# Softmax reciprocals spread through a transpose and transfers from DRAM instead of small matmuls, with the value products dealt out one key tile at a time

## The reference

```python
scores = scale * np.matmul(q, k.transpose(0, 1, 3, 2))
thresh = np.max(scores, axis=-1, keepdims=True) - tau
scores = np.where(scores >= thresh, scores, -1000000000.0)
scores = scores - np.max(scores, axis=-1, keepdims=True)
attn = np.exp(scores)
attn = attn / (np.sum(attn, axis=-1, keepdims=True) + 1e-09)
x = np.matmul(attn, v)                     # then laid out as [tokens, 512]
h = x @ w_in;   x = (h * np.tanh(softplus(h))) @ w_out
h = x @ w_in2;  x = (h * np.clip(h + 3, 0, 6) / 6) @ w_out2
```

## Time and profile before

| | us |
|---|---|
| median of 3 runs (1115.53 to 1116.26) | 1115.55 |
| the profiled execution's own time | 1116.74 |
| its span | 1115.0 |
| PE busy | 1098.8 (99%) |
| DVE busy | 423.6 (38%) |
| ACT busy | 489.9 (44%) |
| POOL busy | 263.5 (24%) |

### The profile page before, as it was taken

The page is one execution under the profiler, slowest core; times in us unless marked ns, Lnnn a source line. Parts: engine busy times, 40 slices in busy tenths (PEclk is TensorE's granted clock), DMA queues, the critical chain, the costliest instruction groups (busy, mean ns, idle before and its releaser), DMA issues.

```text
span 1115.0 us, 15233 instructions
## 1 busy us (share of the span) xinstructions
PE 1098.8 (99%) x6064; PEld 880.3 (79%) x6064; DVE 423.6 (38%) x903; ACT 489.9 (44%) x882; POOL 263.5 (24%) x179
## 2 busy tenths in 40 slices
PE   6999999999999999999999999999999999999998
PEld 5767676767668888889988888888888888888897
DVE  6878887878831211112121112123223223222222
ACT  5778787877743332223232234442233233232232
POOL 6686558556621300000000015430000000000000
PEclk9999999999999999999999999999999999999999
DMA  7432223223022000000000022300010010010010
GB/s 221 132 108 65 77 74 97 65 66 96 11 76 76 1 1 1 1 1 1 1 1 1 19 75 96 96 18 1 1 38 1 1 38 0 1 39 1 1 39 20
DMA packets 42488, 46.09 MB, mean 41 GB/s; under 512 B 3504, under 2 KB 30128, under 8 KB 42416
## 3 DMA queue, kind: packets, MB, share of 16 engines
q1 hardware_dynamic: 42416, 45.10, 13.6%
HBM read 40.37 MB, written 4.72 MB: 40 GB/s over the span
## 4 chain that ended last, share of the span: by engine, by line
PE 97%; DVE 1%; ACT 1%; issue 1%; DMA 0%; SPq 0%; DVEq 0%
PE banks L489 35%; PE banks L462 12%; PE banks L464 12%; PE banks L463 12%; PE banks L409 8%; PE banks L356 7%; PE banks L368 5%; PE banks L364 3%; PE banks L389 2%; DVE probs L709 0%; DVE neg_max L725 0%; ACT exps L572 0%; DMA q_raw<-qT 0%; ACT probsT L537 0%; DVE totals L741 0%
## 5 line engine op out<-in xcount | busy, mean ns | idle before, releaser
L770 DVE SCALAR_TENSOR_TENSOR g_low<-gate,g_high 128x512 fp32r<-128x512 f32 (+1 forms) x160 | 102.7, 642 | 473.2 <-ACT g_high L645 473.2
L462 PE MATMUL banks<-x_low,w_in_high 128*128 128x512 f32 (+1 forms) x640 | 235.9, 369 | 0.0
L463 PE MATMUL banks<-x_high,w_in_low 128*128 128x512 f32 (+1 forms) x640 | 235.5, 368 | 0.0
L464 PE MATMUL banks<-x_high,w_in_high 128*128 128x512 f32 (+1 forms) x640 | 235.5, 368 | 0.0
L645 ACT ACTIVATE g_high<-gate 128x512 fp32r<-128x512 f32 (+1 forms) x160 | 94.3, 589 | 309.6 <-PE banks L489 309.1
L462 PEld LDWEIGHTS banks<-x_low,w_in_high 128*128 128x128 f32 x640 | 120.6, 188 | 21.2 <-issue 0.6
L463 PEld LDWEIGHTS banks<-x_high,w_in_low 128*128 128x128 f32 x640 | 120.6, 188 | 20.5
L464 PEld LDWEIGHTS banks<-x_high,w_in_high 128*128 128x128 f32 x640 | 120.7, 189 | 20.0
L725 DVE TENSOR_REDUCE neg_max<-banks 128x1 f32<-128x576 f32 x144 | 108.7, 755 | 50.3 <-PE banks L356 50.1
L489 PE MATMUL banks<-g_low,w_out_high 128*128 128x512 f32 (+1 forms) x320 | 118.0, 369 | 0.8 <-issue 0.8
L489 PE MATMUL banks<-g_high,w_out_low 128*128 128x512 f32 (+1 forms) x320 | 117.8, 368 | 0.0
(11 more groups left out here) (59 smaller groups left out, 1430.1 us busy)
## 6 DMA issues: line engine op xcount, KB each, us to landing
q_raw<-qT SPq DMA_DIRECT2D x64, 144.0 KB, 2.8
k_raw<-kT SPq DMA_DIRECT2D x64, 144.0 KB, 2.8
w_in_raw<-w_in SPq DMA_DIRECT2D x16, 512.0 KB, 4.3
w_out_raw<-w_out SPq DMA_DIRECT2D x16, 512.0 KB, 4.7
out<-x SPq DMA_DIRECT2D x18, 256.0 KB, 2.9
values<-v SPq DMA_DIRECT2D x16, 256.0 KB, 3.1
values<-v SPq DMA_DIRECT2D x16, 32.0 KB, 2.8
tau_in<-tau SPq DMA_DIRECT2D x1, 0.5 KB, 2.8
```

Of the source, the lines that this page charges most:

```text
L462: nc.tensor.matmul(bank, w_in_high[:, t, cols], low, start=(t == 0), stop=False)
L463: nc.tensor.matmul(bank, w_in_low[:, t, cols], high, start=False, stop=False)
L464: mm = nc.tensor.matmul(bank, w_in_high[:, t, cols], high, start=False, stop=(t == KT - 1))
L770: nc.vector.scalar_tensor_tensor(out=g_low[:, f % 2, 0:width], in0=gate[:, f % 2, 0:width], scalar=1 / 6 if layer_of(c) else 1.0, in1=f32( ...
```

## The change

The spreading matmuls and their copies are gone. In their place PE transposes the pair's 128 x 9 reciprocals once, at `i == 2` (`turn_recips`); ACT copies the 9 x 128 result to `recip_rows` (`keep_recips`); SP stores this to a DRAM row, waits until it has landed, and reads it back in three transfers that lay it out over 64 partitions each (`spread_recips`). DVE's two multiplications wait for these (`spread_loaded`). The key tiles of the value products are dealt to more steps (`part0`, `part1`), DVE's multiplications stand behind `weigh`, and the second is at `i == 2`. The end of the attention is written out by hand.

```diff
+            def spread_recips(pair):
+
+                sp.wait_ge(recip_rows_kept, pair + 1)
+                row = recip_dram[pair % 2]
+                sp.dma_start(row.rearrange("(t p) -> t p", p=P), recip_rows[:, :]).then_inc(recips_stored, 16)
+                sp.wait_ge(recips_stored, 16 * (pair + 1))
+
+                after(sp, x_ready, 2 * pair)
+                sp.dma_start(spread[0:DH, :], row[0:SEQ].partition_broadcast(DH)).then_inc(spread_loaded, 16)
+                sp.dma_start(spread[DH:P, 0:MAIN * P], row[SEQ + TAIL:2 * SEQ].partition_broadcast(DH)).then_inc(spread_loaded, 16)
+                sp.dma_start(spread[DH:P, MAIN * P:SEQ], row[SEQ:SEQ + TAIL].partition_broadcast(DH)).then_inc(spread_loaded, 16)
...
             for k in range(HEADS_IT):
                 load_head(1, k)
+            spread_recips(0)
 
             for it in range(2, ITS):
                 for k in range(HEADS_IT):
                     load_head(it, k)
+                    if k == 1:
+                        spread_recips(2 * it - 3)
                     if k % 2 == 1:
                         load_values(it - 1, k // 2)
+                spread_recips(2 * it - 2)
+            spread_recips(PAIRS - 3)
             for b in range(PAIRS_IT):
                 load_values(ITS - 1, b)
+            spread_recips(PAIRS - 2)
...
                 if g == EARLY_PIECES:
+                    spread_recips(PAIRS - 1)
...
+                    if half == 0 and i == 3:
+
+                        after(pe, recip_rows_kept, t // PAIR_TILES)
...
-            def spread_sums(pair, b, u):
-
-                if u == 0:
-                    pe.wait_ge(recips_ready, pair + 1)
+            def turn_recips(pair, b):
+
+                pe.wait_ge(recips_ready, pair + 1)
+                nc.tensor.transpose(turned_recips[recip_slot(pair)], recips[:, b, :], ident[:, :]).then_inc(recips_turned, 1)
...
-            part0 = {4: (0,), 5: (1, 2), 6: (3, 4)}
-            part1 = {7: (0, 1), 8: (2,), 0: (3,), 1: (4,)}
+            part0 = {3: (0,), 4: (1,), 5: (2,), 6: (3, 4)}
+            part1 = {8: (0,), 0: (1,), 1: (2,), 2: (3, 4)}
...
+            last_pair, last_b = PAIRS - 1, PAIRS_IT - 1
+            up_early(0)
+            mix(ITS, last_pair - 1, 1 - last_b, 1, (1, 2, 3, 4))
+            turn_tail(ITS * TILES_IT - 2, TILES_IT - 2)
+            turn_main(ITS * TILES_IT - 2, TILES_IT - 2)
+            turn_tail(ITS * TILES_IT - 1, TILES_IT - 1)
+            turn_main(ITS * TILES_IT - 1, TILES_IT - 1)
+            turn_recips(last_pair, last_b)
+            up_early(1)
+            up_early(2)
+            mix(ITS, last_pair, last_b, 0, range(MAIN + 1))
+            up_early(3)
+            mix(ITS, last_pair, last_b, 1, range(MAIN + 1))
...
+            def keep_recips(pair):
+
+                act.wait_ge(recips_turned, pair + 1)
+                after(act, recips_stored, 16 * pair)
+                nc.scalar.copy(recip_rows[:, :], turned_recips[recip_slot(pair)]).then_inc(recip_rows_kept, 1)
...
             def scale_mixed(pair, u):
 
+                dve.wait_ge(spread_loaded, 48 * (pair + 1))
                 dve.wait_ge(mixed_ready, 2 * pair + u + 1)
...
-                if i == 6 and (not first or p == 1):
-                    scale_mixed(pair, 0)
-                if i == 1 and not first:
-                    scale_mixed(pair - 1, 1)
                 if (not first or s >= 1) and (ahead or s < 1):
                     weigh(t - 1, (s - 1) % TILES_IT)
+                if ahead and i == 6 and (not first or p == 1):
+                    scale_mixed(pair, 0)
+                if ahead and i == 2 and not first:
+                    scale_mixed(pair - 1, 1)
```

More of the change, by code:

```diff
@@ L116, in attention_and_layers @@
     spread = place("spread", [P, SEQ])
+    recip_rows = place("recip_rows", [PAIR_TILES, P])
     top[0] = shared + (line - shared) % LINE
@@ L142, in attention_and_layers @@
         turned = banks[:, 6, :]
+        turned_recips = [banks[0:PAIR_TILES, 2 * s, BANK - P:BANK] for s in range(3)]
         turned_tail = [banks[:, 2 * s + 1, BANK - P:BANK] for s in range(3)]
@@ L214, in f32, with recip_slot @@
             return ap.bitcast(F32)
+        def recip_slot(pair):
+            return 0 if pair < PAIRS - 1 else 2
         def head_used(it, k):
@@ L398, in mix @@
                     pe.wait_ge(v_loaded[b], 32 * (it + 1 if b == 0 else it))
-                    pe.wait_ge(spread_kept, 2 * pair + 2)
+                    after(pe, x_ready, 2 * pair)
                     pe.wait_ge(main_kept, (pair + 1) * PAIR_TILES)
@@ L426, in attention_step @@
                 if not first or p == 1:
-                    if i in (2, 3):
-                        spread_sums(pair, b, i - 2)
                     if i in part0:
                         mix(it, pair, b, 0, part0[i])
-                    if i in (7, 8):
+                    if i >= 5 and i in part1:
                         mix(it, pair, b, 1, part1[i])
-                if not first and i in (0, 1):
+                if not first and i < 5 and i in part1:
                     mix(it, pair - 1, 1 - b, 1, part1[i])
                 if (not first or s >= 2) and (ahead or s < 2):
-                    turn(t - 2, (s - 2) % TILES_IT)
+                    turn_tail(t - 2, (s - 2) % TILES_IT)
+                    if i == 2 and (not first or p == 1):
+                        turn_recips(pair, b)
+                    turn_main(t - 2, (s - 2) % TILES_IT)
             pe.wait_ge(ident_ready, 1)
@@ L493, in down, with up_early @@
                     mm.then_inc(g_used, 1)
[L496 to L503, removed]
+            def up_early(f):
+                pe.wait_ge(tail_kept, ITS * TILES_IT - 2 + f // 2)
+                up(0, f)
+            last_pair, last_b = PAIRS - 1, PAIRS_IT - 1
[11 more added lines that the diff above has]
+            mix(ITS, last_pair, last_b, 1, range(MAIN + 1))
             pe.wait_ge(main_kept, ITS * TILES_IT)
-            pe.wait_ge(x_ready, 2 * PAIRS)
+            pe.wait_ge(recip_rows_kept, PAIRS)
             for tile in range(STEPS * FT + LAG):
                 c, f = tile // FT, tile % FT
-                if tile < STEPS * FT and not (c == 0 and f in ups_early.values()):
+                if tile < STEPS * FT and not (c == 0 and f < UPS_EARLY):
                     up(c, f)
+                if tile == LAG:
+                    pe.wait_ge(x_ready, 2 * PAIRS)
                 if tile >= LAG:
@@ L561, in attention_step @@
                 first = isinstance(it, int) and it == 0
[L562 to L565, removed]
                 if (not first or s >= 2) and (ahead or s < 2):
                     keep_tail(t - 2, (s - 2) % TILES_IT, it * PAIRS_IT + (s - 2) // PAIR_TILES)
+                if i == 2 and (not first or p == 1):
+                    keep_recips(it * PAIRS_IT + p - 1)
                 if ahead:
@@ L653, in _ @@
                     keep_sums(c - 1)
-                if tile < 2:
-                    attention_step(ITS, tile + 2, ahead=False)
+                if tile == 0:
+                    keep_recips(PAIRS - 1)
                 if layer_of(c):
@@ L742, in attention_step @@
                     dve.wait_ge(totals_ready, pair + 1)
+                    after(dve, recips_turned, pair - 1)
                     nc.vector.reciprocal(recips[:, b, :], totals[:, b, :]).then_inc(recips_ready, 1)
```

29 lines of the change are left out of this document (9 added, 20 removed).

## The result

The changed kernel takes 1197.95 us (median of 4 runs, 1194.81 to 1200.01), the kernel before 1115.64 (4 runs, 1115.53 to 1116.26): ratio 1.0728, 95% interval 1.0708 to 1.0748. So it is 7.3% slower; 1200 had been predicted, in a range of 1178 to 1216. The profiled run took 1194.81, and its mean granted clock is 0.97 instead of 1.00.

What follows compares the result with a forecast made beforehand. It took PE, busy for 99% of the span, to set the pace: 1116.7 - 12.2 + 56.4 + 18.4 + 21 + 0.5 = 1200.8, less 1.2 for the profiled run, say 1200 us; range 1178 to 1216.

Steps and rivals of the forecast that it cites:

- PE's work: Attention, 16 pairs: spreading removed, a transpose and product splits added, a copy awaited; -12.2 us, between -15.4 and -7.4.
- six odd waits, clock included: Iterations 1 to 6: second pair's reciprocals arrive late behind key loads, +56.4 us, plus 3 us each for PE's lower clock.
- first pair, clock included: First pair's store stands behind all four heads of iteration 1: +18.4 us, plus 3 us for PE's lower clock.
- end: End of the attention: the last pair's reads stand behind four `w_out` loads; +0.5 us (-1 to +5).
- the even pairs just make it: Later iterations: even pairs' data come in time only because odd pairs held everything up; cost 0 (0 to 1 each).
- an iteration takes 48 us: Sign to look for in the new profile: attention iterations of 48 us instead of 38.12.
- 16 x 0.76 = -12.2: Attention, per pair: net 0.96 us less on PE, less 0.2 waiting at step 3, so 0.76 saved, 16 times.
- an instruction taken from PE there is worth its whole time: Attention: PE sets the pace, so removed matmul time, 1.44 us per pair, counts in full.
- 3.6 us to spare: Attention, per pair: DVE busy 15.48 of 19.06 us, so it was taken to have this slack.
- the wait: Each odd pair: data 7.0 us after SP is free; PE dry 8.8 us, cost taken as 9.4 (8.8 to 10.1).
- the clock: Behind each of seven long waits PE returns at 1.2 GHz: 3 us each, +21 us in all (0 to 31).
- first rival: The waits come as forecast, but PE returns at 2.4 GHz: 1179 to 1189, say 1182 us; chance 0.2.

Runs made afterwards that it cites:

- E1: The changed kernel with the reciprocals' store and reads moved ahead of the key loads in SP's queue; 1119.9 us, ratio 1.0033 to the kernel before.
- E2: The changed kernel with only the odd pairs' reciprocal transfers moved ahead of the key loads; 1181.03 us, ratio 1.0581.
- E5: The kernel before with the spreading matmuls and their copies left out and nothing in their place; 1111.73 us, ratio 0.9965.
- E4: E1 with the five key tiles of part 1 dealt one each to steps 7, 8, 0, 1 and 2; 1112.91 us, ratio 0.9965.
- E6: E4 with the reciprocals' transpose ahead of step 2's product and ACT's copy of it ahead of the tail's; 1111.58 us, ratio 0.9952.
- E7: E6 with two of eight `w_in` loads ahead of iteration 1's heads, the others one per iteration; 1107.29 us, ratio 0.992.
- E3: The changed kernel with 50 more matmuls of 288 columns ahead of tile 8's scores in iterations 1 to 6; 1192.22 us, ratio 1.068.

## Why the prediction came out, and where it was off

The balance is that of the profiled runs, 1194.81 - 1116.74 = +78.1. The third column is worked out from the table of differences and from E1.

| term | predicted | measured | from |
|---|---|---|---|
| PE's work | -12.2 | about +2.5 | E1: +5.8 when the first layer begins, about 3.3 of it the first pair's (its 3.5 at pair 1 in the table) |
| six odd waits, clock included | 56.4 + 18 | about 59 | period 48.5 us, in E1 38.6 |
| first pair, clock included | 18.4 + 3 | about 16.5 | table, pair 0 |
| end | +0.5 | -0.4 | 803.6 - 804.0 |

**Right:** the place and the cause. The store stands behind the key loads, DVE waits in iterations 1 to 6 and in the first pair, not in iteration 7, the even pairs just make it, and an iteration takes 48 us. E1 and E2 each took away what was claimed, and the time followed.

**Mis-sized, PE's work.** The step "16 x 0.76 = -12.2" failed. Its count was off by one split: only part 0 has one portion more (`part1` has four before and after), so 0.16 and not 0.32, which would have made the term -14.8. But "an instruction taken from PE there is worth its whole time" was false: E5 shows that in the order before the 23 us of spreading are worth 4.5. I had read PE's 19.06 busy of 19.06 as a distance to the other engines, and it says only that none had been late yet; DVE's 15.48 was read as 3.6 us to spare, a mean over the pair that says nothing of one step.

The lengths of PE's steps, means over iterations 2 to 6, show where the saving went. In E1, against the kernel before, step 2 is 1.3 us longer, 0.6 of it more than its matmuls explain (0.4 of that is the wait for the reciprocals' copy at step 3, where 0.2 had been counted). Steps 3 and 5 are 0.3 and 0.4 shorter. Step 7 is 0.6 shorter, though a product of 1.22 left it. And step 8 is 0.6 longer in every second pair, with the same matmuls. The sum is +0.2 per pair.

That last place no run mended: E4, E6 and E7 still have 0.5 there. In step 7 of an iteration's second pair ACT rounds a piece of `w_in`, and its copy of the tail, on which the second half of the next scores waits, stands behind this. ACT and PE in E6:

```profile
153.71 1.06 ACT L618 CAST w_in_high<-w_in_raw 128x1024 fp32r<-128x1024 f32 x1
154.79 0.26 ACT L586 COPY probsT<-banks 64x128 f32<-64x128 f32 x1
```

```profile
155.11 0.40 PE L388 MATMUL banks<-k_high,q_stack 128*128 128x288 f32 x1 [0.20 <-ACT probsT L586]
```

Before, step 7 held two key tiles and lasted 2.45 us, which covered the rounding; now it lasts 1.8 to 1.9. This is read from rows alone.

In another order the term could have come near: E6's 0.59 per pair, 16 times, is 9.4 us, within the bounds of -15.4 to -7.4. What of it is due to DVE's multiplication behind the weighing was not tried by itself.

**Mis-sized, the wait.** PE stood for 7.4 to 7.6 us at each odd pair, 8.8 had been worked out. From SP free to data took 6.2 and not 7.0: the store woke SP after 176.68 - 174.41 = 2.27, where 3.0 had been taken from a transfer of 256 KB as the nearest row, and DVE started 3.84 after that, where 4.0 had been worked out. The other 0.5 is PE, which ran dry 0.3 behind the issue of the key loads and not 0.2 ahead of it (0.1 of this was a slip: 2.4 + 1.2 + 0.7 is 4.3, not 4.2). The Trainium skill, "DMA: Bandwidth & Descriptors", in "Anatomy of one DMA", gives about 2.0 us fixed for a transfer issued by GpSimd, mostly the receipt at its target; the 2.27 for 4.5 KB issued by SP is near to that, but the same store took 1.23 in E1, so the nearness proves nothing (last section).

**Mis-sized, the clock.** The mechanism was right: PE is at 1.2 GHz for 3.5 to 6.7 us behind each wait, and half of that is 1.8 to 3.3 us, in the mean less than the 3 that I had taken. But E3 gives 0.7 to 2.1 where the clock was kept, 1.1 in the mean: PE behind DVE's weighing can't use its full rate at once. The prediction had named this cover only for its first rival ("as DVE's catching up is then covered less") and had not taken it off its own term. Where no long wait follows, a fall seems to cost more: the four executions of E1 with a mean granted clock of 1.000 took 1118.8 to 1119.2 us, the four with 0.997 or 0.998 took 1120.6 to 1122.5, some 2.5 more (only the profiled one shows where it fell, in the first pair).

The time came out 2 us above the median, and 6 above the profiled run (which ran 3 under its median), because the errors cancelled: 15 too low in the work, 20 too high in the waits and the clock, 1 too high at the end. The bounds given to the work term, -15.4 to -7.4, don't hold the +2.5.

What is not settled: 48.5 - 38.6 = 9.9 us per odd wait against 7.5 of standing. By E3 some 1.1 of the 2.4 between them is the clock; the rest I put down to PE behind DVE's weighing and the ordinary fill of the steps again, which was only read from rows, and no run took it apart.

## What to carry to other kernels

Look for the place of a new transfer in its queue before looking at its length: here one wait ahead of it, on an event that has nothing to do with it, cost 78 us, and issuing the same transfers a few lines earlier gave them back. An engine that is busy for 99% is not thereby alone on the path: before a saved instruction is booked at its full time, ask in that very step how far the engine that feeds it is behind. And empty no step of filler work that covered another engine's copy: what the changed order lost in its uneven steps, one product in each step gave back.

## What the runs showed of the hardware

**DVE's small instruction waits for GpSimd's.** `totals` (128 x 9) takes 0.16 us in most places and up to 2.15 in others. In all 16 instances of each of seven kernels (before, after, E1, E4 to E7) it ends 0.02 to 0.04 us behind the GpSimd instruction that was running when it began, and takes 0.16 or 0.17 where none ran or none had more than 0.03 to go. DVE and then GpSimd in the changed kernel:

```profile
371.51 2.14 DVE L776 TENSOR_SCALAR totals<-sums 128x9 f32<-128x9 f32 x1
```

```profile
370.01 3.61 POOL L879 TENSOR_TENSOR x_high<-x,one 128x2048 fp32r<-128x2048 f32 x1
```

370.01 + 3.61 = 373.62, and 371.51 + 2.14 = 373.65. The Trainium skill, "SBUF — State Buffer", in "SBUF: two separate sides", has the two engines share a port pair that the first holds for its whole instruction, where DVE's instruction is in a two-port mode or has two inputs in SBUF; the rows agree for `totals`. The reciprocal behind it, of the same shape, takes 0.21 or 0.22 even while GpSimd works (in the kernel before at 65.07, with 1.31 us of GpSimd's to go). In E1 and E7 DVE loses 0.65 to 0.76 us to this at every second pair, in E5 1.05, in the kernel before mostly nothing, only because there the two instructions miss each other by 0.1 us. In E5 it reaches PE (the 1.01 at 142.22); in E7 the pairs that have it are no longer than the others (18.4 us against 18.6). No run took it away by itself.

**A store's time to its waiter depends on what was issued before it.** The same 4.5 KB store wakes SP after 2.27 us behind two key loads of 144 KB in the changed kernel and after 131.48 - 130.25 = 1.23 in E1, where SP had issued nothing for 7.5 us. Over the changed kernel, E1, E2 and E7 it is 1.22 to 1.28 where SP had issued nothing for 3.7 us or more, and 2.1 to 2.8 where a load of heads or values was issued directly before it.

**The clock can fall after short stands too.** In E1, timeline of PE in the first pair:

```profile
41.03 0.76 PE L425 MATMUL banks<-probsT,values 128*64 128x320 f32 x4 [1.77 <-DVE x L751]
42.55 0.47 PE L396 MATMUL banks<-ident,probs 128*128 128x128 f32 x1 [0.76 <-DVE probs L743]
...
44.22 0.44 PE L388 MATMUL banks<-k_low,q_stack 128*128 128x288 f32 x1
44.46 0.44 PE L388 MATMUL banks<-k_high,q_stack 128*128 128x288 f32 x1
```

The product at 41.03 still ran at 2.4 GHz; behind a wait of 1.77 us and one of 0.76 the matmuls are 0.24 apart, until 50.3 (granted clock 0.58 from 42.55 to 50.30). It need not fall: in E4 PE stood for 2.88 us at the same place, and the granted clock from 41.50 to 48.00 is 1.00.
